# Low-term and maximum part of the transposed scores as 64-row matmul pairs

## The chip, the cores and the metric

The kernel runs on one core of a Trainium2 chip. The metric is the device time of one execution in microseconds (us). A trace of one profiled execution gives every instruction's start and duration. Engines are TensorE (PE; its weight loads are listed apart as PEld), VectorE (DVE), ScalarE (ACT), GpSimd (POOL) and SyncE (SP), which issues the DMAs.

## The reference

Attention on pooled queries, then two feed-forward blocks. 32 heads (4 batches of 8), 1152 keys, 576 pooled queries, head dimension 64.

```python
q_pool = q.reshape(B, H, S // 2, 2, D).mean(axis=3)
scores = scale * np.matmul(q_pool, k.transpose(0, 1, 3, 2))
scores = scores - np.max(scores, axis=-1, keepdims=True)
attn = np.exp(scores)
attn = attn / (np.sum(attn, axis=-1, keepdims=True) + 1e-09)
attn_out = np.matmul(attn, v)
...
h = x @ w_in;  x = (h * sigmoid(h)) @ w_out          # 2304 tokens, 512 -> 2048 -> 512
out = (((x @ w1) * (x @ w2)) @ w3) @ w_out           # 512 -> 1024 -> 1024 -> 512
```

## The kernel before

Every operand of a matmul is split into a high part, rounded to the type fp32r that TensorE multiplies, and a low part, the rest; a product takes two or three matmuls that add up in PSUM. Each engine has its own program, written out by hand, and they meet by semaphores; nothing schedules them.

The attention goes head by head (`h`, with buffer `j` = 0 or 1), in a loop over pairs of heads. A head has nine chunks of 128 keys. In step `s` of a head TensorE does three things, in this order:

- `score_t(h, j, s)`, the transposed scores: keys on the 128 output partitions, 576 queries as two halves of 288 columns, each half in a PSUM bank of its own. Two chunks' worth of banks (`stbank`) alternate; ScalarE takes the exponential of a chunk out of them in one instruction (L516), which `exp_done` reports.
- `score_max` for one to three items of the *next* head: scores with queries on the partitions, 384 keys at a time (L923, L924). VectorE takes the row maximum of each (L708, tile `mx`). Fifteen items make a head; there are two banks for them.
- `values` of the chunk two steps back (`LAG`): two halves of three matmuls of 288 columns (L907 to L909) with `pH` and `pL`, the high and low parts of the exponential, made by ScalarE (L522) and by VectorE (L726) or GpSimd (L424).

In step 7, `turn_max` sits between the two halves of `values`: VectorE has negated the next head's maxima (L717, L719, tile `mneg`), and TensorE turns them into rows with five transposes (L932), four over 128 partitions and a last one over 64. ScalarE puts these two rows (high and low) under the low query terms: `qBs` holds the low part of the queries in partitions 0 to 63 and the two rows of the negated maximum in partitions 64 and 65 (zeros in 66 to 127), and `kB` the high part of the keys in 0 to 63 and ones in 64 to 127. `kA` and `qHs` hold the high and low parts of the keys, and the high part of the queries twice. So one half of the scores, maximum included, is two matmuls:

```python
for a in range(2):
    q = slice(a * HALF, (a + 1) * HALF)
    pe.matmul(out[:, a, :], kA[j][:, keys], qHs[j][:, q], start=True, stop=False)
    last = pe.matmul(out[:, a, :], kB[j][:, keys], qBs[j][:, q], start=False, stop=True)
last.then_inc(st_scored, 1)
```

That is lines 948 and 949. After the attention come the two feed-forward blocks, in tiles of 384 tokens, whose matmuls all have 128 rows.

Of the kernel before, what the change touches and what calls it, by code (L numbers as in the profile page):

```python
# [24 lines left out]
P = 128  # L25


def need(eng, sem, value):

    if isinstance(value, int) and value <= 0:  # L30
        return
    eng.wait_ge(sem, value)


def block_kernel(nc, kT, qT, v, w_in, w_out, w1, w2, w3T, w_out2, ident_in, outT, recips):
    HEADS, D, S = kT.shape
# [11 lines left out]
    NC = S // P  # L48
    HALF = Q // 2
# [22 lines left out]
    with ctx:  # L72
        def sem(name):
            return ctx.enter_context(nc.semaphore(name))


        def sb(name, shape, dt=F32, stack=ctx):
            return stack.enter_context(nc.sbuf_tensor(name, [P] + shape, dt))
# [19 lines left out]
        with ExitStack() as st:  # L98
# [4 lines left out]
            kA = [sb(f"kA{j}", [S], F32R, st) for j in range(2)]  # L103
            kB = [sb(f"kB{j}", [S], F32R, st) for j in range(2)]
            qHm = [sb(f"qHm{j}", [Q], F32R, st) for j in range(2)]
            qLm = [sb(f"qLm{j}", [Q], F32R, st) for j in range(2)]
            qHs = [sb(f"qHs{j}", [Q], F32R, st) for j in range(2)]
            qBs = [sb(f"qBs{j}", [Q], F32R, st) for j in range(2)]
# [75 lines left out]
        m_placed = sem("m_placed")  # L184
        st_scored = sem("st_scored")
        exp_done = sem("exp_done")
        pH_ready = sem("pH_ready")
        pL_dve = sem("pL_dve")
        pL_pool = sem("pL_pool")
# [714 lines left out]
        def _(pe):  # L904
            def three(out, lhs_hi, lhs_lo, rhs_hi, rhs_lo, start, stop):

                pe.matmul(out, lhs_hi, rhs_hi, start=start, stop=False)  # L907
                pe.matmul(out, lhs_hi, rhs_lo, start=False, stop=False)  # L908
                return pe.matmul(out, lhs_lo, rhs_hi, start=False, stop=stop)  # L909
# [26 lines left out]
            def score_t(h, j, c):  # L936

                if c == 0:
                    pe.wait_ge(m_placed, 2 * (h + 1))
                    pe.wait_ge(qHs_ready, h + 1)  # L940
                    pe.wait_ge(qBs_ready, h + 1)
                    pe.wait_ge(kB_ready, KB * (h + 1))
                need(pe, exp_done, NC * h + c - 1)
                keys = slice(c * P, (c + 1) * P)
                out = stbank[(NC * j + c) % 2]
                for a in range(2):
                    q = slice(a * HALF, (a + 1) * HALF)
                    pe.matmul(out[:, a, :], kA[j][:, keys], qHs[j][:, q], start=True, stop=False)  # L948
                    last = pe.matmul(out[:, a, :], kB[j][:, keys], qBs[j][:, q], start=False, stop=True)  # L949
                last.then_inc(st_scored, 1)  # L950

            def values(h, j, c, between=(), turn=None):
# [25 lines left out]
            def pair(i, last):  # L978
                first = isinstance(i, int) and i == 0
                for j in range(2):  # L980
                    h = 2 * i + j
                    more = not (last and j == 1)
                    for s in range(NC):
                        score_t(h, j, s)
                        ahead = [(h + 1, 1 - j, t) for t in items(s)] if more else []

                        at_once = ahead if s in (LAG - 1, LAG) or (first and j == 0 and s < LAG) else ahead[:1]
                        for h_next, j_next, t in at_once:
                            score_max(h_next, j_next, t)
                        if s >= LAG:  # L990
                            values(h, j, s - LAG, ahead[len(at_once):], h + 1 if more and s == NC - 2 else None)
                        elif not (first and j == 0):
                            values(h - 1, 1 - j, NC + s - LAG, ahead[len(at_once):])
# [57 lines left out]
            for c in range(C2):  # L1051
                r = c % 2
                pe.wait_ge(fL_ready, FP * (c + 1))
                for m in FOLD_ORDER:
                    if c == 0 and m == 2:
                        pe.wait_ge(y_taken, TILES * MC)
                    cols = slice(DM + m * P, DM + (m + 1) * P)
                    last = three(psum[:, m, :], fH[r][:, cols], fL[r][:, cols], fH[r][:, 0:DM],
                                 fL[r][:, 0:DM], start=(c == 0), stop=(c == C2 - 1))
# [75 lines left out]
```

## Time and profile before

| | |
|---|---|
| median of two runs | 1468.97 us (1468.89 to 1469.06) |
| span of the profiled execution, first to last instruction | 1465.5 us |
| attention, first turn of the maxima to its last matmul | 21.42 to 716.52 us |
| PE busy over the span | 1352.9 us (92%) |
| DVE, ACT, POOL busy | 799.6, 697.3, 434.8 us |
| granted clock of TensorE, mean | 0.995 of 2.4 GHz |

An engine's busy time is the union of its records. Records of TensorE overlap, because a matmul is still in the array when the next one starts, and the weight load of the next matmul has records of its own (PEld).

### The profile page before, as it was taken

How to read it: one execution, taken by the hardware profiler on the slowest of the kernel's cores; microseconds unless marked ns; L12 is line 12 of the kernel's file. 1: busy time of each engine (PE TensorE's matmuls, PEld its weight loads, DVE VectorE, ACT ScalarE, POOL GpSimd, SP SyncE). 2: the span in 40 equal slices, each digit the busy share in tenths (PEclk: the TensorE clock that was granted, in tenths of full speed). 3: DMA queues.
4: the chain of work that ended last, by engine and by line, in shares of the span. 5: the costliest groups of instructions: out<-in, count | busy, mean ns of one | idle time of the engine just before them, and what ended most of it. 6: DMA issues, size and time to landing. Idle time of an engine off the chain costs nothing.

```text
span 1465.5 us, 24978 instructions
## 1 busy us (share of the span) xinstructions
PE 1352.9 (92%) x8224; PEld 1296.8 (88%) x8224; DVE 799.6 (55%) x1340; ACT 697.3 (48%) x1266; POOL 434.8 (30%) x322
## 2 busy tenths in 40 slices
PE   6888888888888888889999999999999999999998
PEld 5887877787778787778899999999999899999998
DVE  7888888888888889888531111111114522122221
ACT  4776666666666666667742222222224422121211
POOL 4766656666655766655200000000000000000000
PEclk9999999999999999999999999999999999999999
DMA  6233323333323233320220000000104200000000
GB/s 155 73 81 81 95 64 80 81 79 81 91 68 81 68 92 81 79 72 24 61 65 8 1 1 1 1 0 0 43 0 153 92 1 22 23 22 1 21 21 22
DMA packets 33694, 76.34 MB, mean 52 GB/s; under 512 B 8944, under 2 KB 12144, under 8 KB 33648
## 3 DMA queue, kind: packets, MB, share of 16 engines
q1 hardware_dynamic: 33648, 75.73, 19.1%
q8 instruction: 29, 0.48, 0.1%
q14 instruction: 17, 0.14, 0.0%
HBM read 70.84 MB, written 4.79 MB: 52 GB/s over the span
## 4 chain that ended last, share of the span: by engine, by line
PE 77%; DVE 13%; issue 7%; DVEq 1%; DMA 1%; ACT 0%; SPq 0%; ACTq 0%
PE psum L907 21%; PE psum L908 20%; PE psum L909 20%; PE psum L923 5%; PE psum L924 4%; DVE mx L708 4%; PE psum L948 3%; PE psum L949 3%; DVE mneg L717 2%; DVE pL L726 2%; DVE mneg L719 2%; PE psum L932 1%; DVE kB L691 1%; DVE xT L732 1%; DVE qHs L702 1%
## 5 line engine op out<-in xcount | busy, mean ns | idle before, releaser
L708 DVE TENSOR_REDUCE mx<-psum 128x1 f32<-128x384 f32 (+1 forms) x480 | 253.1, 548 | 74.3 <-PE psum L924 73.7
L516 ACT ACTIVATE pF<-psum 128x576 f32<-128x576 f32 x288 | 187.7, 652 | 158.9 <-PE psum L949 156.8
L923 PE MATMUL psum<-kA,qHm 128*128 128x384 f32 (+1 forms) x480 | 172.4, 359 | 60.5 <-DVE mx L708 50.4
L836 DVE TENSOR_TENSOR gL<-gF,gH 128x384 fp32r<-128x384 f32 x96 | 53.6, 558 | 306.0 <-ACT gH L593 306.0
L424 POOL TENSOR_TENSOR pL<-pF,pH 128x576 fp32r<-128x576 f32 x93 | 143.0, 1538 | 216.8 <-ACT pH L522 216.7
L522 ACT CAST pH<-pF 128x576 fp32r<-128x576 f32 x288 | 194.5, 675 | 4.6
L726 DVE TENSOR_TENSOR pL<-pF,pH 128x576 fp32r<-128x576 f32 x195 | 187.6, 962 | 15.0 <-ACT pH L522 14.5
L907 PE MATMUL psum<-pH,vH 128*128 128x288 f32 x576 | 178.7, 310 | 1.5 <-DVE xT L732 0.7
L590 ACT ACTIVATE gF<-psum 128x384 f32<-128x384 f32 x96 | 47.3, 492 | 261.9 <-PE psum L909 261.9
L909 PE MATMUL psum<-pH,vL 128*128 128x288 f32 x576 | 171.0, 297 | 0.0
L908 PE MATMUL psum<-pL,vH 128*128 128x288 f32 x576 | 170.8, 297 | 0.0
L948 PE MATMUL psum<-qHs,kA 128*128 128x288 f32 x576 | 163.7, 299 | 0.8 <-ACT qBs L509 0.8
L949 PE MATMUL psum<-qBs,kB 128*128 128x288 f32 x576 | 163.8, 298 | 0.0
L924 PE MATMUL psum<-kA,qLm 128*128 128x384 f32 (+1 forms) x480 | 163.2, 340 | 0.0
L923 PEld LDWEIGHTS psum<-kA,qHm 128*128 128x128 f32 (+1 forms) x480 | 85.9, 179 | 85.7 <-DVE mx L708 72.0
L883 DVE TENSOR_TENSOR pr<-aS,psum 128x384 f32<-128x384 f32 x48 | 26.6, 555 | 201.0 <-ACT aS L666 201.0
L907 PE MATMUL psum<-gH,woH 128*128 128x384 f32 x384 | 128.4, 334 | 0.4 <-DVE gL L836 0.4
L908 PE MATMUL psum<-gL,woH 128*128 128x384 f32 x384 | 128.3, 334 | 0.0
L909 PE MATMUL psum<-gH,woL 128*128 128x384 f32 x384 | 128.3, 334 | 0.0
L909 PE MATMUL psum<-xH,w12L 128*128 128x384 f32 x384 | 128.3, 334 | 0.0
L909 PE MATMUL psum<-xH,winL 128*128 128x384 f32 x384 | 128.3, 334 | 0.0
L907 PE MATMUL psum<-xH,w12H 128*128 128x384 f32 x384 | 128.3, 334 | 0.0
(88 smaller groups left out, 3030.0 us busy)
## 6 DMA issues: line engine op xcount, KB each, us to landing
qraw<-in_qT SPq DMA_DIRECT2D x64, 288.0 KB, 4.2
kraw<-in_kT SPq DMA_DIRECT2D x64, 288.0 KB, 5.1
vraw<-in_v SPq DMA_DIRECT2D x32, 288.0 KB, 2.7
rsums<-recips SPq DMA_DIRECT2D x32, 144.0 KB, 2.9
outT<-oS SPq DMA_DIRECT2D x6, 768.0 KB, 3.4
wstage<-in_w_in SPq DMA_DIRECT2D x16, 256.0 KB, 3.4
fstage<-in_w3T SPq DMA_DIRECT2D x8, 512.0 KB, 4.7
w12stage<-in_w SPq DMA_DIRECT2D x8, 512.0 KB, 4.7
```

Of the source, the lines that this page charges most:

```text
L424: pool.tensor_tensor(pL[r][:], pF[r][:], pH[r][:].bitcast(F32), ALU.subtract).then_inc(pL_pool, 1)
L516: act.activation(two(pF[r][:]), stbank[(NC * j + c) % 2], ACT.Exp, scale=SCALE).then_inc(exp_done, 1)
L522: act.copy(pH[r][:], pF[r][:]).then_inc(pH_ready, 1)
L708: dve.tensor_reduce(mx[0:m, qt, b:b + 1], max_bank(h, jj, t)[0:m, 0:KW], AX.X, ALU.max)\
L726: dve.tensor_tensor(pL[r][:], pF[r][:], pH[r][:].bitcast(F32), ALU.subtract).then_inc(pL_dve, 1)
L907: pe.matmul(out, lhs_hi, rhs_hi, start=start, stop=False)
L908: pe.matmul(out, lhs_hi, rhs_lo, start=False, stop=False)
L909: return pe.matmul(out, lhs_lo, rhs_hi, start=False, stop=stop)
L923: pe.matmul(out, qHm[jj][:, cols], kA[jj][:, kblock(b)], start=True, stop=False)
L924: pe.matmul(out, qLm[jj][:, cols], kA[jj][:, kblock(b)], start=False, stop=True).then_inc(max_scored, 1)
L948: pe.matmul(out[:, a, :], kA[j][:, keys], qHs[j][:, q], start=True, stop=False)
L949: last = pe.matmul(out[:, a, :], kB[j][:, keys], qBs[j][:, q], start=False, stop=True)
```

## The change

The matmul with `kB` and `qBs` (low query terms and maximum) is no longer one over 128 rows for each half, but two over 64 rows, `upper` (partitions 0 to 63) and `lower` (64 to 127). Each chunk begins with the upper rows for half 0 and the lower rows for half 1, goes on with the two 128-row matmuls of `kA` and `qHs`, and ends with the lower rows for half 0 and the upper rows for half 1. The two matmuls of a pair use different rows of the array and write different banks. A new semaphore, `rows_scored`, is raised by both matmuls of the first pair, and TensorE waits for it before the second pair.

```diff
+        rows_scored = sem("rows_scored")
...
-                for a in range(2):
-                    q = slice(a * HALF, (a + 1) * HALF)
-                    pe.matmul(out[:, a, :], kA[j][:, keys], qHs[j][:, q], start=True, stop=False)
-                    last = pe.matmul(out[:, a, :], kB[j][:, keys], qBs[j][:, q], start=False, stop=True)
+                halves = [slice(a * HALF, (a + 1) * HALF) for a in range(2)]
+                upper, lower = slice(0, D), slice(D, P)
+                for a, rows_of in ((0, upper), (1, lower)):
+                    pe.matmul(out[:, a, :], kB[j][rows_of, keys], qBs[j][rows_of, halves[a]], start=True, stop=False
+                              ).then_inc(rows_scored, 1)
+                for a in range(2):
+                    pe.matmul(out[:, a, :], kA[j][:, keys], qHs[j][:, halves[a]], start=False, stop=False)
+                pe.wait_ge(rows_scored, 2 * (NC * h + c + 1))
+                for a, rows_of in ((0, lower), (1, upper)):
+                    last = pe.matmul(out[:, a, :], kB[j][rows_of, keys], qBs[j][rows_of, halves[a]],
+                                     start=False, stop=True)
                 last.then_inc(st_scored, 1)
```

On TensorE, step 6 of the first head, before: the four matmuls of score_t, then `score_max` (L923, L924) and the first half of `values` (L907 to L909).

```order
L948 MATMUL psum<-qHs,kA 128x288
L949 MATMUL psum<-qBs,kB 128x288
L948 MATMUL psum<-qHs,kA 128x288
L949 MATMUL psum<-qBs,kB 128x288
L923 MATMUL psum<-kA,qHm 128x384
L924 MATMUL psum<-kA,qLm 128x384
L907 MATMUL psum<-pH,vH 128x288
L908 MATMUL psum<-pL,vH 128x288
L909 MATMUL psum<-pH,vL 128x288
```

The same place after (lines are one or more further down: L950 the first pair, L953 the two matmuls over 128 rows, L956 the second pair; L924 and L925 are `score_max`, L908 to L910 `values`).

```order
L950 MATMUL psum<-qBs,kB 128x288 x2
L953 MATMUL psum<-qHs,kA 128x288 x2
L956 MATMUL psum<-qBs,kB 128x288 x2
L924 MATMUL psum<-kA,qHm 128x384
L925 MATMUL psum<-kA,qLm 128x384
L908 MATMUL psum<-pH,vH 128x288
L909 MATMUL psum<-pL,vH 128x288
L910 MATMUL psum<-pH,vL 128x288
```

Six matmuls stand where four stood; those with `kB` now enclose those with `kA`, and nothing else has moved.

## Rows read from the trace of the kernel before

**Rows 1.** The page: the span and the busy time of each engine.

```profile
span 1465.5 us, 24978 instructions
PE 1352.9 (92%) x8224; PEld 1296.8 (88%) x8224; DVE 799.6 (55%) x1340; ACT 697.3 (48%) x1266; POOL 434.8 (30%) x322
```

**Rows 2.** Busy time by stretch: the attention, and what follows it.

```profile
core 0: us, PE busy (x) PEld busy (x) DVE busy (x) ACT busy (x) POOL busy (x), PEclk, DMA share, GB/s
21.42:716.52 695.10, 601.64 (x3970) 556.18 (x3971) 602.62 (x987) 482.59 (x842) 422.48 (x306) 0.99 0.30 76
716.52:1465.00 748.48, 743.37 (x4227) 734.91 (x4225) 181.97 (x322) 208.91 (x415) 1.43 (x1) 1.00 0.08 27
```

**Rows 3.** Timeline of TensorE, 529.79 to 531.34 us: start, duration, line, operation.

```profile
529.79 0.34 PE L923 MATMUL psum<-kA,qHm 128*128 128x384 f32 x1
...
530.14 0.30 PE L907 MATMUL psum<-pH,vH 128*128 128x288 f32 x1
...
531.20 0.30 PE L948 MATMUL psum<-qHs,kA 128*128 128x288 f32 x1
531.34 0.29 PE L949 MATMUL psum<-qBs,kB 128*128 128x288 f32 x1
```

**Rows 4.** Timeline of TensorE: the turns of four heads, with idle time before them.

```profile
524.57 0.22 PE L932 MATMUL psum<-identR,mneg 128*2 128x128 f32 x1 [1.79 <-DVE mneg L719]
...
568.69 0.28 PE L932 MATMUL psum<-identR,mneg 128*2 128x128 f32 x2 [1.79 <-DVE mneg L719]
...
679.50 0.28 PE L932 MATMUL psum<-identR,mneg 128*2 128x128 f32 x2 [0.95 <-DVE mneg L719]
...
698.10 0.28 PE L932 MATMUL psum<-identR,mneg 128*2 128x128 f32 x2
```

**Rows 5.** Groups of TensorE by form, 524.57 to 568.69 us: count, busy, mean.

```profile
L907 PE MATMUL psum<-pH,vH 128*128 128x288 f32 x36 | 11.0, 307 | 0.0
...
L949 PE MATMUL psum<-qBs,kB 128*128 128x288 f32 x36 | 10.1, 295 | 0.0
...
L923 PE MATMUL psum<-kA,qHm 128*128 128x384 f32 x24 | 8.6, 358 | 1.6 <-DVE mx L708 1.6
...
L923 PE MATMUL psum<-kA,qHm 128*64 128x384 f32 x6 | 2.1, 350 | 2.1 <-DVE mx L708 2.1
```

**Rows 6.** TensorE's waits in the attention: us in total, times, longest.

```profile
PE psum L923 <- DVE mx L708: 49.4, 53, 1.5
PE psum L932 <- DVE mneg L719: 44.0, 31, 2.7
```

**Rows 7.** Timeline of TensorE and its weight loads around a turn.

```profile
524.69 0.28 PE L932 MATMUL psum<-identR,mneg 128*2 128x128 f32 x2
524.70 0.08 PEld L932 LDWEIGHTS psum<-identR,mneg 128*2 128x2 f32 x1
524.90 0.08 PEld L932 LDWEIGHTS psum<-identR,mneg 64*2 64x2 f32 x1
525.02 0.19 PEld L907 LDWEIGHTS psum<-pH,vH 128*128 128x128 f32 x1
525.13 0.19 PEld L908 LDWEIGHTS psum<-pL,vH 128*128 128x128 f32 x1
525.02 0.40 PE L907 MATMUL psum<-pH,vH 128*128 128x288 f32 x1
525.26 0.29 PE L908 MATMUL psum<-pL,vH 128*128 128x288 f32 x1
```

**Rows 8.** Timeline of TensorE behind the turn at 435.28 us.

```profile
435.28 0.52 PE L932 MATMUL psum<-identR,mneg 128*2 128x128 f32 x5 [1.79 <-DVE mneg L719]
...
436.13 0.44 PE L908 MATMUL psum<-pL,vH 128*128 128x288 f32 x1
436.37 0.44 PE L909 MATMUL psum<-pH,vL 128*128 128x288 f32 x1
```

**Rows 9.** Busy time by stretch, columns as in rows 2: behind the same turn.

```profile
435.80:437.00 1.20, 1.20 (x5) 1.20 (x6) 1.17 (x2) 1.14 (x3) 0.95 (x1) 0.50 0.29 83
```

## The prediction

> **What bounds the kernel now.** The page comes first [rows 1]: TensorE is busy 92% of the span, VectorE 55%. A share over the whole span hides that the program has two halves, so the next view is the busy time by stage [rows 2]. From 21.42 us, when the first head's maxima are turned, to 716.52 us, the last matmul of the attention, every engine works: TensorE 602 of 695 us, VectorE 603. Behind it (748 us) TensorE is busy 99% and nothing else matters. The change touches only the first half, so the question is how much room TensorE has there.
>
> A busy time of TensorE can't be used for that, since its records overlap: the mean duration of a 288-column matmul is 295 ns in the groups [rows 5], but in the timeline the starts of a run of them lie 0.13 us apart (530.14 to 531.34 is nine steps, 0.133 each), and two steps of 384 columns take 0.35 (529.79 to 530.14), 0.175 each [rows 3]. Start to start is what an instruction costs here. The weight load of the next matmul runs under the present one.
>
> Two heads take 44.12 us (524.57 to 568.69) [rows 4]. The groups of that stretch hold 180 matmuls of 288 columns (five groups of 36) and 60 of 384 (24, 24, 6, 6) [rows 5]: 180 x 0.133 + 60 x 0.175 + about 0.54 for ten transposes = 35.0 us. So 9.1 us in two heads, 4.6 a head, is TensorE not at its rate. What it waits for is VectorE, twice: `mx`, the maxima of the next head, 49.4 us in the stage, and `mneg`, their negation, before the transposes, 44.0 us [rows 6]. Over the stage: 2880 x 0.133 + 930 x 0.175 + 32 x 0.27 = 554 us of 695, which leaves 141 us of room. The last head with maxima shows how little remains when VectorE has less to do: 679.50 to 698.10 is 18.60 us [rows 4] against 17.5 us of work, an excess of 1.1 us.
>
> **The change, part by part.** There are 32 x 9 = 288 chunks. A chunk of score_t has now four matmuls over all 128 rows: 4 x 0.133 = 0.53 us. After it has six: a pair of 64-row matmuls, two of 128 rows, a pair of 64 rows. A 64-row matmul streams the same 288 columns as a 128-row one, so a pair that really runs side by side costs one old matmul, and 1 + 2 + 1 is four again. **Nothing is removed.** At best the count is the same; what is added is the following.
>
> (a) Four changes of the row size per chunk (128 to 64, back, to 64, back). The kernel before has one place where the row size changes: the fifth transpose of a head has 64 rows, behind four of 128 rows and before the 128-row matmuls of `values` [rows 7]. Between equal rows the weight load of the fourth transpose (524.70) starts 0.01 us after the third matmul (524.69). The fourth matmul starts at about 524.75 (a transpose takes 0.22 us [rows 4], and two make a span of 0.28), but the fifth's weight load not until 524.90: 0.15 us later, where 128 columns stream in 0.05 to 0.06 us. So the weight load is not pulled ahead over the change, and waits some 0.10 us beyond the stream. Back to 128 rows it is the same: load at 525.02, 0.12 us behind the load of a matmul of 64 columns. Then that load, 0.11 us (525.02 to 525.13), lies open: the next matmul starts 0.24 us after it instead of 0.13. By these rows a change of row size costs 0.10 (emptying) + 0.11 (open load) less some 0.02 that the normal spacing holds anyway, 0.19 us. All 32 heads have this place. Four per chunk: 0.76 us.
>
> (b) Two more matmuls per chunk, one in each pair. No row of before has two matmuls on different rows. The low bound is 0, both loads and both streams side by side. The high bound is one weight load behind another, 0.11 us each [rows 7]; the stream of the second then runs out 0.11 us after the first, so simultaneous streams would gain almost nothing. Together 0 to 0.22 us. The only row on the matter is the spacing of loads, which speaks for the high end, but it is from loads on the same rows; I take the middle, 0.11, and keep both ends.
>
> The Trainium skill ("TensorEngine Tiling (Array Packing)", Key Properties) says that different tiles can execute weight load and matmul in parallel. By it the term would be 0 and the time that of the low end below, 1579 us. No run here shows it.
>
> (c) The wait on `rows_scored` before the second pair. Behind it on TensorE stand the second pair, then `max` and `values`. It asks for the end of the first pair, and the two 128-row matmuls between must first wait for that pair to leave the array (a), then take 0.11 + 0.13 + 0.22 us themselves. Nothing is left to wait for: 0. Were this cover gone it would cost one emptying, 0.10, which (a) has counted already. The two increments I count at nothing for the same reason.
>
> (d) The order: `kB` and `qBs` are now read first. Both were waited for before the first matmul of a head already; no wait moves. DMA, ScalarE, GpSimd and VectorE keep their instructions.
>
> Sum per chunk: 0.76 + 0.11 = 0.87 us (0.76 to 0.98), times 288: **251 us** more work of TensorE (219 to 282).
>
> **What the room takes of it.** The `mx` waits go: VectorE falls behind in the first steps of a head and has 603 busy us in 695; a head of 22.1 us becomes one of about 26, and it does the same work. For the `mneg` wait, one score_t and half of a `values` stand between the last maximum and the turn, so it shrinks by 0.87 from 1.79 or 0.95 [rows 4]. I take what remains per head as about 0.9 us, near the 1.1 of the head at 679.50: 31 x 0.9 = 28 us of the 141, so 113 are absorbed. Added: 251 - 113 = 138 us. Check by head: 17.5 + 9 x 0.87 + 0.9 = 26.2 us, 4.1 more than 22.1, times 32 is 131. The profiled execution has a span of 1465.5 us and lies 3.5 below the median of 1468.97, which is start and end around the span and stays. 1468.97 + 138 = 1607 us; I say **1607**. Ends of (b): 219 - 109 = 110 gives 1579, 282 - 115 = 167 gives 1636. With the remainder per head between 0.4 and 1.5 us (15 us either way) this case reaches from 1563 to 1652.
>
> **Rivals.** *No emptying, pairs side by side (the time doesn't rise).* If the array took a change of rows without emptying and both loads of a pair together, a chunk would cost 4 x 0.133 again. Place: each score_t; price: 0 to 0.05 us a chunk, up to 14 us of work, half of it in the room: 1469 to 1476. It ends as "not slower" as long as a chunk costs under about 0.25 us more: 72 us of work, of which the stalls on VectorE take over half. For it: rows in the trace stand at transposes alone, which are a special kind. Against: the first of the two changes is between transposes on both sides, and shows 0.15 us. Gain is nearly excluded, as nothing is removed.
>
> The Trainium skill (same page, Theoretical Speedup) gives up to twofold for two row tiles. By it a pair takes the time of one matmul, which is this rival's 1469 us, not a gain, since the split has made two of one.
>
> *No emptying, no overlap.* Six matmuls at 0.133, 0.27 more a chunk: 77 us, of which some 45 vanish in the room: 1500. For it: loads are pulled ahead everywhere else.
>
> *The change does not do what it says:* the pairs run one after the other and each empties too. Then (b) is 0.13 for each of two plus an emptying of 0.10 inside each pair: 0.76 + 0.27 + 0.20 = 1.23, times 288 = 354 us, less 120: 1703.
>
> *The clock.* Behind the turn at 435.28, after an idle 1.79 us, the granted clock was half, 1.2 GHz [rows 9], and the starts were 0.24 us apart instead of 0.13 [rows 8]. Over the attention it is 0.99 [rows 2], and the same idle time before 524.57 and 568.69 [rows 4] brought no such stretch; with the stalls filled, the longest idle should shrink. If the small gaps within chunks brought it for good, 17.5 us of work a head would be over 30, and the time beyond 1900.
>
> **How the numbers follow.** Emptying, 1563 to 1652: 0.77, on both sides of which 0.03 lies just outside. Not slower, 1469 to 1497: 0.07. Six in a row, about 1500: 0.05. Emptying within pairs, about 1700: 0.05. The clock: 0.02. Faster by over 2%: 0.01. The likeliest is the first, and the range of 8 in 10 is its own, with some slack: 1560 to 1656. A measurement here tells 2%, 29 us, from no change; the chances are 0.01 faster, 0.07 within, 0.92 slower.
>
> **What the profile after would show.** (a) weight loads of the first 64-row matmul and of the first 128-row one behind it at 0.2 us or more after the previous start, in every chunk; if they stand 0.13 after it, (a) is wrong. (b) the distance between the starts of a pair's two loads: near 0, or 0.11; if over 0.2, the pairs don't overlap. (c) no TensorE idle put down to its own matmuls. The room: waits on `mx` near zero, on `mneg` under 1 us a head, head to head 25.5 to 27 us. The stage behind the attention should keep its 748 us; if it doesn't, or the clock row shows under 0.98 in the attention, the sum is wrong in a place I have not priced.

## The result, and the profile after

The changed kernel takes **1575.76 us** (1575.00 and 1576.51) against 1468.97: ratio 1.0726, 95% interval 1.0709 to 1.0743. It is 107 us slower. By stage, with the columns of [rows 2]:

```profile
core 0: us, PE busy (x) PEld busy (x) DVE busy (x) ACT busy (x) POOL busy (x), PEclk, DMA share, GB/s
21.48:824.23 802.75, 793.65 (x4545) 596.99 (x4546) 556.88 (x987) 486.42 (x842) 390.54 (x306) 0.99 0.25 66
824.23:1573.00 748.77, 743.36 (x4227) 734.90 (x4225) 182.01 (x322) 208.64 (x415) 1.43 (x1) 1.00 0.08 27
```

The attention has grown from 695.10 to 802.75 us, which is the whole difference; the feed-forward stage kept its 748. The granted clock is as it was. VectorE, as busy as TensorE before (603 us), has 557 busy us now.

One chunk in the timeline, first the weight loads, then the matmuls; L950 is the first pair, L953 the two 128-row matmuls, L956 the second pair:

```profile
560.38 0.19 PEld L910 LDWEIGHTS psum<-pH,vL 128*128 128x128 f32 x1
560.74 0.18 PEld L950 LDWEIGHTS psum<-qBs,kB 64*128 64x128 f32 x2 [0.17 <-issue]
561.07 0.30 PEld L953 LDWEIGHTS psum<-qHs,kA 128*128 128x128 f32 x2
561.53 0.19 PEld L956 LDWEIGHTS psum<-qBs,kB 64*128 64x128 f32 x2 [0.17 <-issue]
561.86 0.19 PEld L924 LDWEIGHTS psum<-kA,qHm 128*128 128x128 f32 x1
```

```profile
560.52 0.29 PE L910 MATMUL psum<-pH,vL 128*128 128x288 f32 x1
560.74 0.40 PE L950 MATMUL psum<-qBs,kB 64*128 64x288 f32 x2
561.07 0.53 PE L953 MATMUL psum<-qHs,kA 128*128 128x288 f32 x2
561.53 0.40 PE L956 MATMUL psum<-qBs,kB 64*128 64x288 f32 x2
561.86 0.44 PE L924 MATMUL psum<-kA,qHm 128*128 128x384 f32 x1
562.14 0.34 PE L925 MATMUL psum<-kA,qLm 128*128 128x384 f32 x1
```

The last matmul of `values` starts at 560.52. The loads of the first pair don't follow under it, but at 560.74, 0.22 us later: about 0.12 us of streaming (the 0.133 between two starts holds little else) and 0.10 in which no new load begins. What the array does in this 0.10 us no trace shows; it is called emptying here, as in the prediction. Then **two loads of a pair, merged in one row, span 0.18 us, what one alone takes**: in all 288 first pairs of the trace the second load starts 2 to 5 ns behind the first. From a pair's loads to the next load it is 0.33 us in both pairs (560.74 to 561.07, 561.53 to 561.86): one open load (0.11), one stream (0.12), one emptying (0.10). That second matmul is free. From 560.52 to the start of L924's stream (0.175 before 562.14, so 561.96) it is 1.44 us, where five steps of 0.133 were 0.67 [rows 3]: 0.78 us a chunk more, 222 us in 288 chunks.

Of the waits of [rows 6] one is gone and the other a quarter:

```profile
PE psum L933 <- DVE mneg L720: 10.3, 31, 2.7
PE psum L950 <- ACT qBs L510: 0.8, 1, 0.8
```

and the turns stand 25.11 us apart (44.12 for two heads before, [rows 4]), somewhat under the 25.5 to 27 us that were forecast:

```profile
549.20 0.28 PE L933 MATMUL psum<-identR,mneg 128*2 128x128 f32 x2 [0.26 <-DVE mneg L720]
...
574.31 0.28 PE L933 MATMUL psum<-identR,mneg 128*2 128x128 f32 x2 [0.26 <-DVE mneg L720]
```

### The profile page after: what moved, and what is told of

Read it like the earlier page. It is cut to its first block, busy times and chain, and to the rows that moved or that the text cites. A ratio compares the mean times of both kernels' runs of the same rounds, so it can differ in the third digit from the quotient of the medians.

```text
span 1573.2 us, 26186 instructions
## 1 busy us (share of the span) xinstructions
PE 1545.1 (98%) x8800; PEld 1338.2 (85%) x8800; DVE 753.8 (48%) x1340; ACT 700.8 (45%) x1266; POOL 402.8 (26%) x322
## 4 chain that ended last, share of the span: by engine, by line
PE 93%; DVE 5%; issue 1%; DMA 0%; ACT 0%; SPq 0%; DVEq 0%
PE psum L908 21%; PE psum L909 20%; PE psum L910 20%; PE psum L924 8%; PE psum L953 8%; PE psum L950 5%; PE psum L956 5%; PE psum L925 5%; DVE mneg L718 3%; DVE mx L709 1%; PE psum L933 1%; DMA kraw<-in_kT 0%; DVE mneg L720 0%; DVE mcol L715 0%; DVE rpacked L738 0%
## 5 line engine op out<-in xcount | busy, mean ns | idle before, releaser
L709 DVE TENSOR_REDUCE mx<-psum 128x1 f32<-128x384 f32 (+1 forms) x480 | 258.1, 551 | 207.7 <-PE psum L925 206.1
L425 POOL TENSOR_TENSOR pL<-pF,pH 128x576 fp32r<-128x576 f32 x93 | 131.8, 1417 | 315.7 <-ACT pH L523 315.7
L924 PE MATMUL psum<-kA,qHm 128*128 128x384 f32 (+1 forms) x480 | 184.0, 383 | 10.7 <-DVE kA L752 9.7
L727 DVE TENSOR_TENSOR pL<-pF,pH 128x576 fp32r<-128x576 f32 x195 | 182.6, 936 | 21.2 <-ACT pH L523 20.6
L908 PE MATMUL psum<-pH,vH 128*128 128x288 f32 x576 | 180.5, 313 | 0.7 <-DVE pL L727 0.5
L909 PE MATMUL psum<-pL,vH 128*128 128x288 f32 x576 | 170.0, 295 | 0.0
L910 PE MATMUL psum<-pH,vL 128*128 128x288 f32 x576 | 169.4, 294 | 0.0
L925 PE MATMUL psum<-kA,qLm 128*128 128x384 f32 (+1 forms) x480 | 164.3, 342 | 0.0
L953 PE MATMUL psum<-qHs,kA 128*128 128x288 f32 x576 | 153.7, 349 | 0.0
L908 PE MATMUL psum<-gH,woH 128*128 128x384 f32 x384 | 128.4, 334 | 0.3 <-DVE gL L837 0.3
L910 PE MATMUL psum<-xH,winL 128*128 128x384 f32 x384 | 128.3, 334 | 0.0
L909 PE MATMUL psum<-xL,winH 128*128 128x384 f32 x384 | 128.3, 334 | 0.0
L908 PE MATMUL psum<-xH,w12H 128*128 128x384 f32 x384 | 128.3, 334 | 0.0
L909 PE MATMUL psum<-gL,woH 128*128 128x384 f32 x384 | 128.3, 334 | 0.0
L910 PE MATMUL psum<-xH,w12L 128*128 128x384 f32 x384 | 128.3, 334 | 0.0
L909 PE MATMUL psum<-xL,w12H 128*128 128x384 f32 x384 | 128.3, 334 | 0.0
L908 PE MATMUL psum<-xH,winH 128*128 128x384 f32 x384 | 128.3, 334 | 0.0
L910 PE MATMUL psum<-gH,woL 128*128 128x384 f32 x384 | 128.3, 334 | 0.0
```

What stands on the lines that cost most here:

```text
L425: pool.tensor_tensor(pL[r][:], pF[r][:], pH[r][:].bitcast(F32), ALU.subtract).then_inc(pL_pool, 1)
L709: dve.tensor_reduce(mx[0:m, qt, b:b + 1], max_bank(h, jj, t)[0:m, 0:KW], AX.X, ALU.max)\
L727: dve.tensor_tensor(pL[r][:], pF[r][:], pH[r][:].bitcast(F32), ALU.subtract).then_inc(pL_dve, 1)
L924: pe.matmul(out, qHm[jj][:, cols], kA[jj][:, kblock(b)], start=True, stop=False)
L925: pe.matmul(out, qLm[jj][:, cols], kA[jj][:, kblock(b)], start=False, stop=True).then_inc(max_scored, 1)
L953: pe.matmul(out[:, a, :], kA[j][:, keys], qHs[j][:, halves[a]], start=False, stop=False)
```

## The experiments

Two theories stood at the start: A, the cost is the emptying of the array at each change of row size; B, it is the greater number of matmuls, or the wait on `rows_scored`. Each run was timed beside the kernel before on the same chip (medians 1468.7 to 1469.6). A version of the changed kernel without the wait wasn't tried: the wait is what keeps the two pairs, which use different rows, from writing one bank at the same time. That it costs nothing where it stands is read from the timeline: the second pair's loads start 0.22 us behind the start of the matmul ahead of them, and so do the first pair's, which have no such wait.

**Six whole matmuls.** All over 128 rows, wait and increments kept:

```diff
-                for a, rows_of in ((0, upper), (1, lower)):
-                    pe.matmul(out[:, a, :], kB[j][rows_of, keys], qBs[j][rows_of, halves[a]], start=True, stop=False
+                for a in range(2):
+                    pe.matmul(out[:, a, :], kB[j][:, keys], qBs[j][:, halves[a]], start=True, stop=False
...
-                for a, rows_of in ((0, lower), (1, upper)):
-                    last = pe.matmul(out[:, a, :], kB[j][rows_of, keys], qBs[j][rows_of, halves[a]],
+                for a in range(2):
+                    last = pe.matmul(out[:, a, :], kB[j][:, keys], qBs[j][:, halves[a]], start=False, stop=True)
```

> Six matmuls a chunk as in the changed kernel, with its wait and its increments, but all over 128 rows, so no change of row size (the product with kB is added twice, so the scores are not the reference's). Theory A, the cost lies in emptying the array at each change of row size: only 2 x 0.133 = 0.27 us of work more a chunk than before, 77 us in all, of which the stalls on VectorE take more than half: 1490 to 1505 us. Theory B, the cost is the greater number of matmuls or the wait on rows_scored: at least the 1576 us of the changed kernel.

Measured: 1483.41 us, ratio 1.0098 (1.0081 to 1.0115). B is out as the cause of the 107 us: with the same number of matmuls and the same wait, but no change of row size, 93 of the 107 us are not there. Of 77 us of added work the room took 63, more than I allowed. Its waits show where from:

```profile
PE psum L933 <- DVE mneg L720: 31.9, 31, 3.2
PE psum L924 <- DVE mx L709: 5.2, 14, 0.4
```

The `mx` waits, 49.4 us before, are all but filled.

**Pairs on the same rows.**

```diff
-                for a, rows_of in ((0, upper), (1, lower)):
+                for a, rows_of in ((0, upper), (1, upper)):
...
-                for a, rows_of in ((0, lower), (1, upper)):
+                for a, rows_of in ((0, lower), (1, lower)):
```

> The changed kernel with both matmuls of a pair on the same 64 rows (first pair upper, upper; second lower, lower). Nothing else differs: four changes of row size a chunk, six matmuls. Theory A with pairs that run side by side: without different rows the second matmul of each pair costs its 0.13 us again, with TensorE the bound all of it shows: 1576 + 288 x 0.27 = 1652 us. Rival, the pairs are not what makes the loads start together: 1576 us as it was.

Measured: 1641.99 us, ratio 1.1170 (1.1151 to 1.1189), 66 us over the changed kernel. In the timeline the load after the pair comes 0.46 us behind the pair's first, not 0.33, and the two loads span 0.29, not 0.18:

```profile
562.02 0.29 PEld L950 LDWEIGHTS psum<-qBs,kB 64*128 64x128 f32 x2 [0.17 <-issue]
562.48 0.30 PEld L953 LDWEIGHTS psum<-qHs,kA 128*128 128x128 f32 x2 [0.16 <-issue]
```

So different rows are what lets a pair run side by side, and that is worth 0.13 us a pair: 576 pairs, 75 us, of which 66 showed. Of the other 9, 7 went into the wait for `mneg`, 10.3 us in the changed kernel; here one wait of 3.2 is left.

**Six changes of row size.** The second 64-row matmul comes behind the first 128-row one:

```diff
                 for a, rows_of in ((0, upper), (1, lower)):
                     pe.matmul(out[:, a, :], kB[j][rows_of, keys], qBs[j][rows_of, halves[a]], start=True, stop=False
                               ).then_inc(rows_scored, 1)
-                for a in range(2):
                     pe.matmul(out[:, a, :], kA[j][:, keys], qHs[j][:, halves[a]], start=False, stop=False)
```

> The order in a chunk is 64, 128, 64, 128 rows, then the second pair: six changes of row size instead of four, and the first two 64-row matmuls no longer neighbours. Theory A: two more changes at 0.19 us and one matmul at 0.13 us that no longer runs beside another, 0.51 us a chunk, 147 us: 1723 us. Theory B, the count of matmuls or the wait, gives the 1576 us of the changed kernel.

Measured: 1712.29 us, ratio 1.1661 (1.1640 to 1.1682). A is right in size:

```profile
560.11 0.18 PEld L950 LDWEIGHTS psum<-qBs,kB 64*128 64x128 f32 x1
560.44 0.19 PEld L952 LDWEIGHTS psum<-qHs,kA 128*128 128x128 f32 x1
560.77 0.19 PEld L955 LDWEIGHTS psum<-qBs,kB 64*128 64x128 f32 x2
561.10 0.19 PEld L924 LDWEIGHTS psum<-kA,qHm 128*128 128x128 f32 x1
```

Between two changes of row size a matmul of 288 columns takes 0.33 us instead of 0.133, whether it has 64 rows or 128, and whether it is one or a pair. My sum gave 11 us too much. The wait for `mneg`, still 10.3 us in the changed kernel and 2.7 here, took up 7 or 8 of them; the rest isn't traced.

**Two changes, the wait uncovered.** The 128-row matmuls come first, then both pairs with the wait between them:

```diff
+                for a in range(2):
+                    pe.matmul(out[:, a, :], kA[j][:, keys], qHs[j][:, halves[a]], start=True, stop=False)
                 for a, rows_of in ((0, upper), (1, lower)):
-                    pe.matmul(out[:, a, :], kB[j][rows_of, keys], qBs[j][rows_of, halves[a]], start=True, stop=False
+                    pe.matmul(out[:, a, :], kB[j][rows_of, keys], qBs[j][rows_of, halves[a]], start=False, stop=False
                               ).then_inc(rows_scored, 1)
-                for a in range(2):
-                    pe.matmul(out[:, a, :], kA[j][:, keys], qHs[j][:, halves[a]], start=False, stop=False)
```

> A chunk begins with its two 128-row matmuls, then both pairs of 64-row matmuls one behind the other, with the wait on rows_scored between them: two changes of row size a chunk instead of four, but the wait has no cover. Theory A: 2 x 0.19 us saved would be 109 us, but the second pair must wait until the first has ended and its semaphore is seen, and its loads lie open: 0.39 us for the first pair's record and 0.04 for the semaphore before the second pair's loads, against 0.33 from pair to next load in the changed kernel. Added over the kernel before: 0.69 us a chunk instead of 0.77, so 1550 to 1560 us. Rival, the change of row size is all: 0.38 us a chunk, 109 us of work, mostly in the room: under 1510 us.

Measured: 1569.36 us, ratio 1.0688 (1.0670 to 1.0705), 9 us over the upper end expected.

```profile
562.63 0.19 PEld L952 LDWEIGHTS psum<-qBs,kB 64*128 64x128 f32 x2 [0.17 <-issue]
563.12 0.19 PEld L956 LDWEIGHTS psum<-qBs,kB 64*128 64x128 f32 x2 [0.30 <-PE psum L952]
563.44 0.19 PEld L924 LDWEIGHTS psum<-kA,qHm 128*128 128x128 f32 x1
```

From the first pair's loads to the second's it is 0.49 us, not 0.43: here a wait of TensorE on its own last matmul costs 0.16 us more than a change of row size in the same place (0.49 against 0.33). The first pair's record lasts 0.40 us, and the next loads start 0.09 us after its end, where 0.04 was reckoned. With two changes fewer and this wait instead, the kernel gains 6 us of the 107. The changed kernel's place for the wait, under the two 128-row matmuls, was the cheap one, as (c) had it.

**Only the odd chunks split.** In score_t, `if c % 2 == 1:` the new order, `else:` the old one.

> Only the four odd chunks of each head are split, 128 of 288; the other five are as before. It measures the room. Work added 128 x 0.77 = 98 us. If the stalls on VectorE give way first, they take some 70 of it: 1495 to 1505 us. If the room takes the same share of each microsecond as in the whole change, 107 x 128 / 288 = 47 us: 1516 us.

Measured: 1481.55 us, ratio 1.0091 (1.0074 to 1.0108). The room took 85 of the 98 us, more than either expectation. Put together (work added by the timelines, time added by the medians):

| kernel | work added, us | time added | into the room |
|---|---|---|---|
| six whole matmuls | 77 | 14 | 63 |
| odd chunks | 98 | 13 | 85 |
| the change | 222 | 107 | 115 |
| pairs on the same rows | 222 + 75 = 297 | 172 | 125 |
| six changes | 288 x 1.31 = 377 | 243 | 134 |

(The 1.31 is the 0.78 of the change, plus two more stretches of 0.33, less one of 0.133.) Added work of up to 98 us is nearly free; from the change to the last row, 155 us of work bring 136 of time. The full room was put at 141.

**The place in the kernel before where the row size changes.** If A holds, the fifth transpose of a head costs there too. Over 128 rows, its upper half zeros of unused queries:

```diff
                 for qt in range(QT):
-                    m = rows(qt)
+                    m = P
```

> The kernel before with its fifth transpose of a head over 128 rows as the other four; its rows 64 to 127 hold the zeros of unused queries, and their columns are not read. No matmul of the program changes the row size any more. Theory A: two changes a head less, some 0.09 us before the transpose and 0.17 behind it, less 0.03 for 64 more columns, about 0.2 us a head on the path behind the wait for mneg, 32 times: 5 to 7 us faster, 1462 to 1464 us. Theory B, the row size costs nothing and the gap at the transposes is their own: 1469 to 1470 us.

Measured: 1452.84 us, ratio 0.9882 (0.9866 to 0.9899), and in a second series (below) 1455.12 us, 0.9896 (0.9878 to 0.9913). **This version is 1.1% faster than the kernel before.** That is a small step, but its interval is clear of 1 in both series. The turn is shorter as foreseen: from the first transpose to the second matmul behind it 0.48 us, where it was 0.69 [rows 7]:

```profile
560.21 0.46 PE L932 MATMUL psum<-identR,mneg 128*2 128x128 f32 x5 [1.79 <-DVE mneg L719]
560.50 0.35 PE L907 MATMUL psum<-pH,vH 128*128 128x288 f32 x1
560.69 0.30 PE L908 MATMUL psum<-pL,vH 128*128 128x288 f32 x1
```

That is 32 x 0.21 = 7 us; the gain is 14 to 17. So I made the turn long again without a change of row size:

```diff
+                for _ in range(3):
+                    last = pe.transpose(maxbank[1][0:2, 0:P].bitcast(F32R), mneg[:, QT - 1, :], identR[:])
                 last.then_inc(m_turned, 1)
```

> The kernel with its fifth transpose over 128 rows, with that transpose done three more times into the same place: no change of row size, but some 0.17 us more for the turn, so that it lasts about as long as in the kernel before. If the gain of that kernel (16.8 us, where 0.2 us a head are 6) comes from the length of the turn alone, this one runs as the kernel before, 1467 to 1470 us. If the length explains only its 6 us and the rest comes from how the work of VectorE and GpSimd falls together, 1455 to 1465.

> The kernel with its fifth transpose over 128 rows once more, on the same chip as the one with three transposes more: 1450 to 1457 us as before.

Measured: 1453.74 us with the three transposes more, ratio 0.9897 (0.9880 to 0.9914), the same as without them, though the turn takes 0.67 us again:

```profile
512.99 0.47 PE L932 MATMUL psum<-identR,mneg 128*2 128x128 f32 x5 [1.78 <-DVE mneg L719]
...
513.66 0.30 PE L908 MATMUL psum<-pL,vH 128*128 128x288 f32 x1
```

**My reason for this gain fell**: it isn't the length of the turn. Three more runs, on whether it is the missing changes or a shift of the engines against each other: the old turn with its first transpose done twice, done five times (`for qt in [0] * 4 + list(range(QT))`), and the new one with six more.

> The kernel before, with the first transpose of a head done twice: 0.06 us more for the turn, its two changes of row size kept. If the two changes themselves cost the 15 us that the kernels without them gained, 1469 to 1472 us. If what was gained comes from which operations of VectorE and GpSimd fall together, and any small shift can change that, the time may land anywhere from 1450 to 1475, not in proportion to the shift.

> The kernel before, with the first transpose of a head done five times: 0.23 us more for the turn, its two changes of row size kept. If the changes themselves cost the 15 us: 1473 to 1480 us. If the fall of VectorE's and GpSimd's operations decides: anywhere from 1450 to 1480.

> The kernel with all transposes over 128 rows and six more of them, 0.35 us longer than without: no change of row size, and longer than the turn of the kernel before. If the absence of the changes is what gains: 1455 to 1460 us. If the fall of the operations decides: anywhere up to 1475.

Measured, with what the profiles say of TensorE's granted clock in these runs:

| kernel | runs | median, us | ratio (95%) | lowest and highest, us | clock, same two runs |
|---|---|---|---|---|---|
| before | 19 | 1469.20 | | 1466.10, 1471.87 | 0.996, 0.993 |
| first transpose twice | 10 | 1469.01 | 0.9998 (0.9988 to 1.0007) | 1467.59, 1470.85 | 0.994, 0.992 |
| first transpose five times | 10 | 1463.23 | 0.9974 (0.9948 to 0.9999) | 1458.70, 1471.78 | 0.989, 0.981 |
| all over 128 rows, six more | 6 | 1459.35 | 0.9953 (0.9935 to 0.9972) | 1449.64, 1465.47 | 0.998, 0.984 |

A turn that was made *longer*, changes kept, got faster in six of ten runs. The spread of 13 to 16 us in the last two rows, where the kernel before spreads over 6, goes with the granted clock: nearly without exception, the slower run has the lower clock. An estimate from these numbers: 0.008 of a span of 1465 us is 12 us of TensorE's time, and the two runs in the third row differ by 13. In the profiled run of that kernel (1458.85 us) the clock is half in nine stretches of the attention, for instance from 561.00 to 562.00 us, behind an idle 1.78 us before the turn at 558.57; in the kernel before it is half in four, one of them that of [rows 9]. Even so four of its ten runs took 1459 us, 10 under the median of the kernel before, at a lower clock and with both changes of row size. So a gain of 10 us, where the kernels without the changes have 14 to 17, can be had with the changes in place.

VectorE's operations change their length too. In the heads from 21.4 to 680 us, before, and with the fifth transpose whole:

```profile
L697 DVE CAST qBs<-qLm 64x576 fp32r<-64x576 f32 x30 | 30.6, 1019 | 0.0
L719 DVE SCALAR_TENSOR_TENSOR mneg<-mcol,mneg 128x5 fp32r<-128x5 f32 x30 | 22.2, 740 | 1.0
```

```profile
L697 DVE CAST qBs<-qLm 64x576 fp32r<-64x576 f32 x31 | 22.3, 718 | 0.0
L719 DVE SCALAR_TENSOR_TENSOR mneg<-mcol,mneg 128x5 fp32r<-128x5 f32 x30 | 32.5, 1084 | 1.0
```

One got shorter, the other longer, with the same work; over the attention VectorE was busy 603 us; with the fifth transpose whole it is 593 (up to 706 us), and 573 with the first done five times. What fixes the pattern, and how the gain divides between the shorter turn, the missing changes and the pattern, stays open; the two kernels without changes and with at most three transposes more were the only ones steadily at 1450 to 1457.

**66 rows instead of 64.** Does any change of row count cost this, or only some? The kernel before, with its `kB` matmuls over the 66 rows that hold something:

```diff
-                    last = pe.matmul(out[:, a, :], kB[j][:, keys], qBs[j][:, q], start=False, stop=True)
+                    last = pe.matmul(out[:, a, :], kB[j][0:D + 2, keys], qBs[j][0:D + 2, q], start=False, stop=True)
```

> The kernel before with its matmuls of kB and qBs over the 66 rows that hold something (low terms and the two rows of the maximum) instead of 128; order and number unchanged. If the array empties at any change of the number of rows, each such matmul stands between two changes, four a chunk at 0.19 us: 1575 us or more. If it empties only where the array is divided (64 rows or fewer), nothing changes: 1468 to 1471 us.

Measured: 1469.04 us, ratio 1.0006 (0.9997 to 1.0016). The loads are pulled ahead as between equal rows; each starts with the matmul before it:

```profile
561.00 0.29 PE L948 MATMUL psum<-qHs,kA 128*128 128x288 f32 x1
561.00 0.19 PEld L949 LDWEIGHTS psum<-qBs,kB 66*128 66x128 f32 x1
```

Alternation of 66 and 128 rows, four times a chunk, is free; that of 64 and 128 costs 0.19 to 0.20 us each time.

## Why the prediction was right

The forecast was 1607 us in a range of 1560 to 1656; measured are 1575.76. The case (emptying at each change) and the direction held; the point was 31 us too high, and one term of the sum explains it.

- **Nothing is removed**: right. Side by side, a pair takes the place of one matmul, and 1 + 2 + 1 is four.
- **(a) four changes at 0.19 us, 0.76 a chunk**: right; the timeline gives 0.78 for the whole chunk. The five transposes of a head, an unusual place, priced an ordinary matmul well, and in the new trace the sign set for (a) stands in every chunk: the next load starts 0.22 us or more after the start of the matmul before it. The six-changes run confirms it per change, the six whole matmuls show that little else costs.
- **(b) 0.11 us for the pairs' second matmuls**: mis-sized; it measured 0 to 0.02. I had taken the middle between no cost and one load behind the other, because the only spacing of loads on record, 0.11 us, was from loads on the same rows. With different rows they start together. That is 0.11 x 288 = 32 us of a miss of 31: (a) came out about 3 us higher, so the work is 222 us and not 251, and the room took 2 us more. The low end by rows, 1579, had it. The Trainium skill ("TensorEngine Tiling (Array Packing)", Key Properties) stated this, that tiles can load and multiply in parallel, and the trace agrees: two loads in 0.18 us, where two on the same rows take 0.29. The twofold speedup that the same page gives for two row tiles (Theoretical Speedup) can't help here, as the pairs were made by splitting.
- **(c) the wait is free where it stands**: right. Uncovered it costs 0.16 us over an emptying, not nothing as I wrote there ("which (a) has counted already"); the semaphore's way came on top.
- **The room, 113 of 141 us**: the sum came out (115), by a reason that was partly wrong, so the agreement is in part luck. I held VectorE's work constant and left 0.9 us a head. In fact its busy time fell by 46 us: `mneg`'s second step, 0.74 us on average before, takes 0.17 now, and the `kB` casts 0.37 instead of 0.65; the wait for `mneg` that was left is 0.3 us a head, not 0.9. I had also not seen how lopsided the room is: with 98 us of work added, 85 vanish.
- **The rivals**: no emptying is excluded by the timeline and by six whole matmuls, which cost 14 us where the split costs 107; emptying within pairs by the 0.33; the clock stayed at 0.99.

## What to carry to other kernels

A pair of 64-row matmuls on different rows costs what one matmul costs, so a split by rows can gain only if it makes fewer such passes than before; that is reasoned from these prices, no run here had fewer. Against it stands 0.2 us at each change between 64 and 128 rows: gather the matmuls of one row size, but not so that one pair has to wait for the one just ahead of it, which took back all but 6 us here. Where a short last tile has 64 rows among 128-row work, fill it up to the full size, or use a few rows over 64 where there are any: at the turn that saved 0.21 us each time, and alternating 66 and 128 rows cost nothing. Before pricing more work on an engine that waits, measure how much of it vanishes; here 85 of 98 us vanished, and 115 of 222. And when runs of one kernel spread, look at the granted clock of each before looking for another cause.

## What the runs showed of the hardware that was not expected

- Two weight loads on different 64 rows run together (0.18 us for both); on the same rows the second starts 0.11 us later.
- Alternating 66 and 128 rows is as good as 128 throughout (1469.04 us), without the gap at the change. So not every change in the number of rows costs something: 128 to 64 does, 128 to 66 doesn't.
- A change in the number of stationary columns doesn't cost it either. In the changed kernel `score_max` has matmuls of 64 stationary columns (128\*64) ahead of others of 128, and the next load is pulled ahead as usual, in nine of ten such places within 4 ns of the start of the matmul before:

```profile
559.32 0.34 PE L925 MATMUL psum<-kA,qLm 128*64 128x384 f32 x1
```

```profile
559.32 0.19 PEld L924 LDWEIGHTS psum<-kA,qHm 128*128 128x128 f32 x1
```

- VectorE's short operations have two lengths in these traces. In the changed kernel, from 21.4 to 800 us:

```profile
L692 DVE CAST kB<-kraw 64x384 fp32r<-64x384 f32 x93 | 34.1, 369 | 0.0
L720 DVE SCALAR_TENSOR_TENSOR mneg<-mcol,mneg 128x5 fp32r<-128x5 f32 x31 | 5.1, 166 | 1.1
```

  In the kernel before, the same step at 567.32 lasts 1.32 us, under a subtraction of GpSimd that starts at 567.21 and ends at 568.61:

```profile
567.32 1.32 DVE L719 SCALAR_TENSOR_TENSOR mneg<-mcol,mneg 128x5 fp32r<-128x5 f32 x1
```

```profile
567.21 1.40 POOL L402 TENSOR_TENSOR qLm<-qsum,qHm 128x576 fp32r<-128x576 f32 x1
```

  It is so all through that trace. Of its 32 such steps 15 start while this subtraction runs; they last 1.31 to 1.32 us, and each ends 0.02 us after it. The 17 that start with no GpSimd operation under way last 0.17. The `kB` casts take 0.34 us where none is under way (64 of 96), 1.25 on average where one is. In the changed kernel no `mneg` step of this kind and 4 of the 96 casts start under one. That the one holds up the other is read from these times; no run took GpSimd's work away to show it. The Trainium skill ("GPSIMD Engine Reference", Specifications) says that GpSimd's SBUF interfaces are shared with VectorE, with contention for VectorE's instructions of two SBUF inputs among others, and this step has two; the trace agrees with that, and adds the price, 1.32 us for a step of 0.17.
- A kernel's time can hang on such coincidences: repeating one transpose four times more made its median 1463 instead of 1469 us. It also brought the granted clock down to half more often, which spread the runs over 13 us.
